# Removing three small pads between the activation buffers of an attention and two-MLP kernel

## The reference

```python
qn = q / (norm(q, axis=1) + 1e-6);  kn = k / (norm(k, axis=1) + 1e-6)
s = kn.transpose(0, 2, 1) @ qn / tau          # 256 x 256 per batch, contraction over 6016 rows
a = exp(s - max(s));  a /= sum(a) + 1e-9
x = (v @ a).reshape(12032, 256)
x = (sigmoid(x @ w_gate) * (x @ w_val)) @ w_out     # d_ff = 1536
h = x @ w_in                                        # d_ff = 2048
out = (h - tanh(h)) @ w2_out
```

## Time and profile before

| | |
|---|---|
| median of 3 runs | 2388.05 us (2379.46 to 2388.67) |
| the profiled execution | 2385.13 us, of which the span is 2383.3 us |
| TensorE busy | 2348.7 us, 99% of the span |
| weight loads busy | 1937.0 us, 81% |
| VectorE, ScalarE, GpSimd busy | 49%, 39%, 4% |
| mean granted TensorE clock | 0.995 of 2.4 GHz |

### The profile page before, as it was taken

One profiled execution on the slowest core, in us unless ns is written; L12 is line 12 of the kernel. 1 busy time (PEld: TensorE's weight loads), 2 busy tenths in 40 slices (PEclk: granted clock), 3 DMA queues, 4 the chain that ended last, 5 costly groups with the idle time before them and its releaser, 6 DMA issues.

```text
span 2383.3 us, 28301 instructions
## 1 busy us (share of the span) xinstructions
PE 2348.7 (99%) x10332; PEld 1937.0 (81%) x10332; DVE 1161.8 (49%) x1643; ACT 936.3 (39%) x1550; POOL 106.3 (4%) x76
## 2 busy tenths in 40 slices
PE   8899999999999999999989999999999999999998
PEld 6778888888888888888888888888888888888888
DVE  6965445445354454453554544544445445445344
ACT  5544334334344343343433433433434434334343
POOL 3440000000000000000130000000000000000000
PEclk9999999999999999999999999999999999999999
DMA  9620000100100001001110000010010000100000
GB/s 312 217 62 7 12 9 9 18 9 9 18 9 9 16 2 18 9 7 18 29 42 16 3 15 9 9 18 9 9 18 9 9 12 6 18 9 7 9 9 7
DMA packets 211649, 61.81 MB, mean 26 GB/s; under 512 B 200224, under 2 KB 200480, under 8 KB 211616
## 3 DMA queue, kind: packets, MB, share of 16 engines
q1 hardware_dynamic: 208304, 49.31, 9.3%
q0 software_dynamic: 3312, 12.06, 1.6%
HBM read 49.02 MB, written 12.32 MB: 26 GB/s over the span
## 4 chain that ended last, share of the span: by engine, by line
PE 94%; DVE 2%; POOL 1%; issue 1%; DMA 1%; ACT 0%; SPq 0%; DVEq 0%; ACTq 0%
PE up L755 55%; PE acc L755 22%; PE x_acc L755 17%; DMA qk_in<-in_k 1%; PE x_acc L781 1%; DVE sq_sum L539 1%; POOL in_w_lo L385 0%; POOL out_w_lo L385 0%; ACT squares L402 0%; POOL in_w_hi L383 0%; SPq L297 0%; DVE vt_lo L630 0%; POOL out_w_hi L383 0%; DVE g_lo L654 0%; POOL w_stage L363 0%
## 5 line engine op out<-in xcount | busy, mean ns | idle before, releaser
L447 ACT ACTIVATE func_out<-up 128x512 f32<-128x512 f32 (+1 forms) x672 | 395.9, 589 | 853.1 <-PE up L755 852.9
L654 DVE TENSOR_TENSOR g_lo<-product,g_hi 128x512 fp32r<-128x512 f32 (+1 forms) x672 | 469.2, 698 | 397.2 <-ACT g_hi L455 393.9
L455 ACT ACTIVATE g_hi<-product 128x512 fp32r<-128x512 f32 (+1 forms) x672 | 418.6, 623 | 445.8 <-PE acc L755 220.4
L645 DVE TENSOR_TENSOR product<-up,func_out 128x512 f32<-128x512 f32 (+1 forms) x288 | 196.4, 682 | 473.5 <-ACT func_out L447 473.2
L648 DVE TENSOR_TENSOR product<-up,func_out 128x512 f32<-128x512 f32 (+1 forms) x384 | 261.4, 681 | 193.3 <-ACT func_out L447 184.3
L755 PE MATMUL up<-x_lo,in_w_hi 128*128 128x512 f32 (+1 forms) x768 | 299.6, 390 | 1.0 <-DVE x_lo L637 1.0
L755 PE MATMUL up<-x_hi,in_w_hi 128*128 128x512 f32 (+1 forms) x768 | 300.1, 391 | 0.0
L755 PE MATMUL up<-x_hi,in_w_lo 128*128 128x512 f32 (+1 forms) x768 | 298.6, 389 | 0.0
L755 PE MATMUL acc<-g_hi,out_w_lo 128*128 128x512 f32 (+1 forms) x768 | 297.0, 387 | 0.0
L755 PE MATMUL acc<-g_hi,out_w_hi 128*128 128x512 f32 (+1 forms) x768 | 296.4, 386 | 0.0
L755 PE MATMUL acc<-g_lo,out_w_hi 128*128 128x512 f32 (+1 forms) x768 | 296.2, 386 | 0.0
(11 more groups left out here) (122 smaller groups left out, 2309.8 us busy)
## 6 DMA issues: line engine op xcount, KB each, us to landing
v_in<-in_v SPq DMA_DIRECT2D x176, 64.0 KB, 2.2
out_rows<-out_sb SPq DMA_DIRECT2D x176, 64.0 KB, 1.8
qk_in<-in_q SPq DMA_DIRECT2D x29, 384.0 KB, 4.0
qk_in<-in_k SPq DMA_DIRECT2D x29, 384.0 KB, 4.8
w_stage<-in_moe_w_out POOLq DMA_DIRECT2D x4, 512.0 KB, 4.2
w_stage<-in_moe_w_gate POOLq DMA_DIRECT2D x3, 512.0 KB, 6.0
out_sb<-in_moe_w_val POOLq DMA_DIRECT2D x3, 512.0 KB, 5.8
out_sb<-in_moe_w_out POOLq DMA_DIRECT2D x3, 512.0 KB, 4.3
```

Source lines behind the costliest of these rows:

```text
L447: act.activation(func_out[:, half, cut], src[:, cut], func).then_inc(func_made, 1)
L455: act.activation(hi[:, i % SLOTS, cut], product[:, half, cut], ACT.Copy).then_inc(g_hi_made, 1)
L645: dve.tensor_tensor(product[:, half, cut], up[2 * (i % 2) + 1][:, cut], func_out[:, half, cut], ALU.mult).then_inc(prod_made, 1)
L654: dve.tensor_tensor(lo[:, i % SLOTS, cut], product[:, half, cut], hi[:, i % SLOTS, cut].bitcast(F32), ALU.subtract).then_inc(g_lo_made, 1)
```

## The change

The three pads are taken away. `g1`, `x2` and `g2` then begin 64, 128 and 256 bytes earlier, and all four activation pairs begin at the same place as the weights, modulo 512 bytes. The small `tau_inv` behind them moves by 256 bytes too. No instruction, wait or order on any engine changes: on PE, DVE, ACT, POOL and SP the programs of before and after are the same list, with other addresses.

```diff
         func_out = sb("func_out", [P, 2, T])
         product = sb("product", [P, 2, T])
         vt_hi, vt_lo = pair("vt", [P, KC, T])
-        sb("pad_g1", [P, 16])
         g1_hi, g1_lo = pair("g1", [P, SLOTS, T])
-        sb("pad_x2", [P, 16])
         x2_hi, x2_lo = pair("x2", [P, KC, T])
-        sb("pad_g2", [P, 32])
         g2_hi, g2_lo = pair("g2", [P, SLOTS, T])
         tau_inv = sb("tau_inv", [P, 2])
```

## The result

The change makes the kernel faster: 2349.87 us (median of 4 runs, 2343.44 to 2354.47) against 2388.36 us, a ratio of 0.9844 with a 95% interval of 0.9826 to 0.9861. That is 38.5 us. The forecast was 2393 us with a range down to 2375, so it missed in size and in sign.

The account below looks back on a forecast made before the run. TensorE, busy 99% of the span, was taken as the bound: matmul count times pitch. Terms of +7.6 - 2.1 + 0 + 0 = +5.5 us on 2388.05 gave 2393.5 us, range 2375 to 2420.

Parts of the forecast that it names:

- the clean one: Lowest matmul pitch in the profile, 226.7 ns for 512 columns; the kernel stood 3.9 ns above it, 38 us in all.
- U: Matmuls streaming `vt`, 0 bytes from the weights' place, read at 230.8 ns; their addresses stay, so no gain was forecast.
- the O term: Matmuls streaming `g2`, moved from 256 to 0 bytes: 2304 x 3.3 ns = +7.6 us, bounds 0 and +11.5.
- P: Matmuls streaming `x2`, moved from 128 to 0 bytes: 2304 x (-0.9) ns = -2.1 us, bounds -11.5 and +9.4.
- D: Matmuls streaming `g1`, moved from 64 to 0 bytes: forecast 0, bounds -8.6 and +7.1 us.
- the first fold: Early matmuls at 0 bytes reading 226.7 ns, used for the lower bound of 0 on the price of that place.
- The later fold: Later matmuls at 0 bytes reading 231.7 ns, used for the upper bound of 5.0 ns on that place's price.
- The faster one: Rival: offsets of 64 and 128 bytes cost, so D and P gain 20.1 us; 2368 us, chance 0.10.
- Nothing moves: Rival: the excess pitch comes from alternating operands and banks, not from place; 2388 us, chance 0.25.
- The place adds: Rival: both streams collide at equal places, 6336 x 4.1 ns = +26.0 us on top; 2414 us, chance 0.35.
- ACT, DVE and the waits: Operations on `g` and `x2` at moved addresses: nothing to gain or lose, 0 us, and no growth in TensorE's waits.

## Why the prediction was wrong, point by point

**The bound and the frame were right.** The time is the number of matmuls times the pitch. The 38 us between the pitch before and the clean one were named as all that any placement could give back, and the change gave back all of it.

**The step that failed** is the reading of each kind's pitch as the property of its own place. U at distance 0 read 230.8 ns, and this was taken as the price of that distance, both for the O term (+7.6 us) and to hold P and D where they were. U's distance costs nothing: its 4.1 ns is what it pays for following D at another place, and it went when D moved, at operands that the change left alone. That U might gain was in no term of the sum; its 3456 matmuls x 4.1 ns are 14.2 us by this one chunk, and 13.2 of the 38.9 us by all chunks of the ten tiles.

**The clue was in the rows.** O at a tile's end and the first fold were clean, and a chunk just behind another kind was not. I put O's extra 3.3 ns between chunks of P down to ACT's read of PSUM or to the switch of operands and said that it stays. It was the switch of places: in the changed kernel the read is there as before and O is clean. The later fold, 231.7 ns at distance 0, was used as the upper bound for a price of that distance. It stands behind matmuls of 256 columns and a gap, and reads the same in the changed kernel, (124.78 - 123.39) / 6 = 231.7 ns. That fits the passing cost behind a change of width, shown above, but no run moves the fold away from its neighbours.

**Term by term.** O: forecast +7.6, measured (226.7 - 230.0) over its steady 13 of 16 chunks, 1872 x (-3.3) = -6.2 us. P: forecast -2.1, measured 2304 x (-5.0) = -11.5 us, the lower bound given for it. D: forecast 0, measured 1728 x (-5.0) = -8.6 us, its lower bound too. U: no term, measured -14.2 us. The sum, -40.5, is within the reading error of the 38.9 us of the chain, since each term rests on one chunk. Added up by kind from the starts of all 4080 matmuls of the ten tiles, times 2.4, the gain is O 4.4, P 13.1, D 8.2 and U 13.2 us, together 38.9: P gave a little more than its bound.

**How much is distance, how much change?** From the steady pitches, D at 64 bytes is worth 720 x 2.22 ns = 1.6 us in ten tiles and P at 128 bytes 960 x 5.71 ns = 5.5 us. The remaining 9.1 of 16.2 us, 22 of 39 us in all, are changes of place. This split assumes that D and P pay their steady price in full while alternating, which no run shows apart; P's chunks between O's average 231.9 ns, a little under the steady 232.4, so the two costs don't simply add.

**The rivals.** The faster one had the sign, and the right drop for D and P (20 us), but was given 0.10: its counter-argument, that U and the later folds at 0 are not clean, was the same misreading. "Nothing moves" was also the result by the rule of the Trainium skill, "TensorE: Matmul & The Clock Gate", section "Step-by-step: what each phase is for", that TensorE has two independent read ports and a weight load takes no read bandwidth from the running matmul. What the prediction drew from it, that the pitch doesn't depend on the distance, doesn't hold here: it runs from 226.67 to 233.33 ns for these fp32r operands, and the measurement decides. Whether the streams meet at the ports, no run shows. "The place adds" was wrong in sign: in the steady chunks nothing is paid at equal places.

**ACT, DVE and the waits** behaved as forecast: 623 ns as before, and TensorE's wait for `g_lo` 6.4 us instead of 6.7.

**What stays open.** The runs show that distance and change of place cost, not why. Which unit delays the streams, what is carried over for some ten matmuls behind a change of place or of width, and why a distance of 32 costs three times what 64 does, none of them tells.

## What to carry to other kernels

Where TensorE's matmuls run back to back and are the bound, line up the starts of stationary and moving operands modulo 256 bytes, for all the products that alternate; a small odd-sized buffer allocated in between cost 0.7 to 2.6% here. This is measured for fp32r operands with a weight load ahead of each matmul of 512 columns; other types and other ratios of loads to matmuls were not run. Read the pitch from starts over whole tiles, where 0.01 us is visible, not from durations. And a slow stretch may be paying for its neighbour: before a pitch is taken as the price of a stretch's own layout, look for the same layout beside other neighbours, and for changes of width ahead of it.

## What the runs showed of the hardware

- The pitch of fp32r matmuls of 512 columns, each with its own weight load, takes fixed values by the distance of the two operands in SBUF, the same for all four kinds: 226.67 ns at 0 and 256 bytes, 228.89 at 64 and 320, 232.38 at 128, 233.33 at 32 and at 448, each from ten tiles of one trace. The two pairs 256 bytes apart, 0 and 256, 64 and 320, are equal.
- A change of place by 64 bytes between neighbouring products costs about 48 ns for each chunk of 18 matmuls with two such changes, even when both operands change together; a change by 256 bytes costs nothing.
- A change from 384 to 512 columns, with every operand at one place, is followed by six matmuls at 231.7 ns and six more at 228.3 to 230.0 ns before the clean pitch comes back (the changed kernel; shown from 1260.69 us).
- The ACT and DVE operations beside the matmuls (0.6 to 0.7 us each) leave the clean pitch alone: with the same ACT and DVE work as before, ten tiles take 924.80 us, 226.67 ns for each matmul, the lowest pitch in any of these runs.
